# A chunked recurrence on one core: inverse decays by one reciprocal, inputs loaded in three parts, preparation seven slots ahead

## What is computed

```python
for t in range(S):
    y[:, :, t] = np.einsum('bhd,bhde->bhe', rt, state)
    Sa = np.einsum('bhde,bhe->bhd', state, at)
    state_decay = state * wt[:, :, None, :] - np.einsum('bhd,bhe->bhde', Sa, bt)
    state = state_decay + np.einsum('bhd,bhe->bhde', vt, kt)
```

## Time and profile before

| | us |
|---|---|
| median of 3 executions | 1002.68 |
| lowest, highest | 999.1, 1007.23 |
| the profiled execution | 1005.59 |
| its span in the trace | 1003.9 |
| TensorE busy in the span | 826.9 |
| VectorE busy in the span | 556.5 |

### The profile page before, as it was taken

How to read it: one execution, slowest core, us unless ns; L and a number is a source line. 1 busy time by engine, 2 the same in 40 slices (tenths; PEclk the granted TensorE clock), 3 DMA queues, 4 the chain that set the end, 5 groups by cost and what they waited for, 6 DMA issues and landing times.

```text
span 1003.9 us, 27604 instructions
## 1 busy us (share of the span) xinstructions
PE 826.9 (82%) x11872; PEld 603.9 (60%) x11872; DVE 556.5 (55%) x1235; ACT 312.4 (31%) x739; POOL 252.2 (25%) x524
## 2 busy tenths in 40 slices
PE   2318988897998978859998789997899987899977
PEld 2218888897887978844454555455544545554555
DVE  8686667767776653125436635347355366353464
ACT  3102222223222222212225532235422255312354
POOL 1075856687776876000000000000000000000000
PEclk9999787898777888789999999999999999999999
DMA  3525455565656536232000000100000000000000
GB/s 102 137 57 115 96 131 127 131 147 112 137 121 132 133 73 159 60 101 81 10 31 7 21 14 1 40 1 21 14 7 30 10 12 17 14 1 0 1 21 20
DMA packets 125336, 61.31 MB, mean 61 GB/s; under 512 B 105120, under 2 KB 118048, under 8 KB 123296
## 3 DMA queue, kind: packets, MB, share of 16 engines
q1 hardware_dynamic: 95172, 32.61, 14.5%
q10 hardware_dynamic: 30044, 26.94, 10.4%
HBM read 45.37 MB, written 14.16 MB: 59 GB/s over the span
## 4 chain that ended last, share of the span: by engine, by line
PE 66%; DVE 15%; DMA 7%; ACT 6%; issue 4%; SPq 2%; ACTq 1%; DVEq 0%
PE ps_all L737 9%; PE ps_all L721 8%; PE ps_scan L103 4%; PE ps_all L778 4%; DMA l_by_unit<-l_blocks 3%; PE ps_all L854 3%; PE ps_all L815 3%; PE ps_scan L194 3%; ACT probs L914 3%; PE ps_scan L174 3%; PE ps_all L833 3%; PE ps_all L731 3%; PE ps_all L845 2%; PE ps_all L724 2%; DVE t_update_first L314 2%
## 5 line engine op out<-in xcount | busy, mean ns | idle before, releaser
L314 POOL TENSOR_TENSOR t_update<-l_by_unit,t_by_unit 128x133 f32<-128x133 f32 (+13 forms) x251 | 118.0, 470 | 131.8 <-DVE t_by_unit L316 64.4
L316 POOL TENSOR_TENSOR t_by_unit<-t_by_unit,t_update 128x133 f32<-128x133 f32 (+13 forms) x251 | 128.8, 513 | 19.7
L103 PE MATMUL ps_scan<-decayed_a_and_eye,scaled_then_x 40*128 40x104 f32 x768 | 67.8, 346 | 55.9 <-DVE decayed_a_and_eye L346 55.9
L721 PE MATMUL ps_all<-scaled_then_x,inputs_then_w_up 128*128 128x384 f32 x256 | 91.0, 499 | 15.7 <-DMA scaled_then_x<-y_t 10.0
L103 PEld LDWEIGHTS ps_scan<-decayed_a_and_eye,scaled_then_x 40*128 40x128 f32 x768 | 62.7, 252 | 57.9 <-DVE decayed_a_and_eye L346 42.3
L1005 DVE TENSOR_REDUCE minus_max<-ps_all 128x1 f32<-128x128 f32 (+5 forms) x96 | 54.9, 618 | 75.2 <-PE ps_all L819 75.2
L737 PE MATMUL ps_all<-gated,w_down 128*128 128x384 f32 x256 | 91.1, 499 | 0.0
L721 PEld LDWEIGHTS ps_all<-scaled_then_x,inputs_then_w_up 128*128 128x128 f32 x256 | 48.7, 194 | 52.2 <-issue 12.0
L880 ACT ACTIVATE h<-ps_all 128x384 f32<-128x384 f32 x64 | 28.0, 490 | 148.7 <-PE ps_all L724 148.7
L737 PEld LDWEIGHTS ps_all<-gated,w_down 128*128 128x128 f32 x256 | 46.0, 189 | 44.6 <-issue 19.1
L951 DVE TENSOR_SCALAR conv<-h,w_conv 128x768 f32<-128x768 f32 x32 | 19.9, 621 | 94.7 <-ACT h L880 94.7
(11 more groups left out here) (115 smaller groups left out, 1519.2 us busy)
## 6 DMA issues: line engine op xcount, KB each, us to landing
inputs_then_w_up<-in_x ACTq DMA_DIRECT2D x46, 321.4 KB
r_t_and_v_t<-in_rv ACTq DMA_DIRECT2D x48, 160.0 KB
l_by_unit<-l_blocks SPq DMA_DIRECT2D x24, 256.0 KB, 5.0
uv_and_ruv<-in_v ACTq DMA_DIRECT2D x48, 80.0 KB, 3.0
y_t<-y_out SPq DMA_DIRECT2D x24, 160.0 KB
out<-out_rows SPq DMA_DIRECT2D x24, 160.0 KB, 1.8
l_blocks<-ak_and_l SPq DMA_DIRECT2D x96, 32.0 KB, 2.0
t_blocks<-t_by_unit SPq DMA_DIRECT2D x24, 128.0 KB, 4.7
```

Source lines behind the costliest of these rows:

```text
L103: last = nc.tensor.matmul(PS[:, o:o + ROWS], weights, AL[c % NK][rows(h), p, :], start=True, stop=True)
L314: return (lambda: eng.tensor_tensor(tmp[:, 0:cols, 0:rest], l[:, s:s + 1, s + 1:BLK].broadcast_to(shape), t[:, 0:cols, s:s + 1].broadcast_ ...
L316: lambda: eng.tensor_tensor(t[:, 0:cols, s + 1:BLK], t[:, 0:cols, s + 1:BLK], tmp[:, 0:cols, 0:rest], ALU.subtract))
L721: nc.tensor.matmul(bank[n][:, 0:HALF], WIN[:, t, cols], XT[:, t, n * HALF:(n + 1) * HALF], start=(t == 0), stop=False)
```

## The change

Four things change together. (1) `suffixes`, a small reciprocal and a backward scan, becomes `inverses`: one reciprocal of all 104x512 prefix products into a new tile; the tiles of the scan go. (2) The load of a chunk is cut in three: w, then a, then k and b, each with its semaphore; 46 load DMAs become three times as many, each of a part. w of chunk n+8 is loaded after the first move of slot n, a of chunk n+7 after the second, k and b of chunk n+8 after bkn_move. (3) GA goes from 6 to 7: one slot more before slot 0, an eighth `decayed_a_and_eye`, `ak_and_l` and `bk_natural`, a ninth `prefix_products`. (4) The order within a slot: in odd slots with a head VectorE begins with four steps of the head, then hm, then five steps, then gm, and only then prefixes and inverses; ScalarE does the second x move ahead of bkn_move. solve_first stands in slot -3, again behind gm of chunk 3.

```diff
--- before.py
+++ after.py
@@ -20,11 +20,13 @@
 WCOLS = P8 * SEGW
 HC = P8 * C
 XCOLS = WCOLS + 1 + 3 * HC
-GA = 6
+GA = 7
 NK = GA + 1
 NQK = GA + 2
 NPAIR = NT // 2
 HEAD = 9
+FIRST = 4
+PARTS = {"w": slice(0, WCOLS + 1), "a": slice(WCOLS + 1, WCOLS + 1 + HC), "kb": slice(WCOLS + 1 + HC, XCOLS)}
 
 
 def recurrence(nc, sem, in_x, in_v, in_rv, l_dram, t_dram, y_t, inputs, scaled, load_weights, load_tokens):
@@ -35,9 +37,8 @@
     INX = [inputs[0:ROWS, n * XCOLS:(n + 1) * XCOLS] for n in range(2)]
     BK = [scaled[0:ROWS, n * 2 * HC:(n + 1) * 2 * HC].rearrange("r (p j t) -> r p j t", p=P8, j=2) for n in range(2)]
     PF = [sb(f"prefix_products{n}", [ROWS, WCOLS]) for n in range(NQK)]
-    SF = sb("suffix_products", [ROWS, WCOLS + 3])
+    IV = sb("inverse_products", [ROWS, P8, C])
     ONE = sb("reset_ones", [ROWS, WCOLS + 1])
-    RST = sb("reset_inverses", [ROWS, WCOLS + 1])
     AL = [sb(f"decayed_a_and_eye{n}", [ROWS, P8, ROWS]) for n in range(NK)]
     GM = [sb(f"ak_and_l{n}", [128, 2, P8, C]) for n in range(NK)]
     BKN = [sb(f"bk_natural{n}", [128, 2, P8, D]) for n in range(NK)]
...
@@ -244,11 +245,11 @@
                 act.wait_ge(m["t_out"], 32 * (j - 1))
             nc.scalar.activation(TS[j % 2][:, :, :], EYE[:, :, :], ACT.Copy).then_inc(m["eye"], 1)
 
-        def load_x(c):
+        def load_x(c, part):
             if c >= 2:
                 act.wait_ge(m["prepped"], c - 1)
             for h in range(2):
-                act.dma_start(INX[c % 2][rows(h), :], in_x[c, h]).then_inc(m[f"inx{c % 2}"], 16)
+                act.dma_start(INX[c % 2][rows(h), PARTS[part]], in_x[c, h][:, PARTS[part]]).then_inc(m[f"{part}{c % 2}"], 16)
 
         def load_v(n):
             if n >= 3:
@@ -264,7 +265,8 @@
                               in_rv[n, h].rearrange("r k p t -> r (k p t)")).then_inc(m[f"r{n % 3}"], 16)
 
         act.wait_ge(m["set_inx"], 2)
-        load_x(1)
+        for part in ("w", "kb", "a"):
+            load_x(1, part)
         act.wait_ge(m["consts"], 4)
         for n in range(NK):
             for h in range(2):
@@ -277,11 +279,14 @@
         for n in range(-GA, NT + 1):
             c = n + GA - 1
             live, ahead = 0 <= n < NT, 0 <= c < NT
+            soon, next_up = 2 <= n + GA < NT, 2 <= n + GA + 1 < NT
             if live: move(XS, PX, "x", "x_sb", n)
+            if next_up: load_x(n + GA + 1, "w")
             if live: move(YS, PY, "y", "y_sb", n, -1.0)
-            if 2 <= n + GA + 1 < NT: load_x(n + GA + 1)
+            if soon: load_x(n + GA, "a")
+            if live: move(ZS, PX, "e", "z_sb", n)
             if ahead: bkn_move(c)
-            if live: move(ZS, PX, "e", "z_sb", n)
+            if next_up: load_x(n + GA + 1, "kb")
             if live: u_move(n)
             if live:
                 act.wait_ge(m["st"], n + 1)
@@ -319,27 +324,25 @@
     def vector(dve):
 
         def prefixes(c):
-            dve.wait_ge(m[f"inx{c % 2}"], 32 * (c // 2 + 1))
+            dve.wait_ge(m[f"w{c % 2}"], 32 * (c // 2 + 1))
             if c >= 1:
                 dve.wait_ge(m["prepped"], c)
             link(dve, nc.vector.tensor_tensor_scan(PF[c % NQK][:, :], INX[c % 2][:, 0:WCOLS], ONE[:, 0:WCOLS], 0.0,
                                                    ALU.mult, ALU.add))
 
-        def suffixes(c):
-            ends = RST[:, 1:WCOLS + 1].rearrange("r (p w) -> r p w", w=SEGW)[:, :, C]
-            link(dve, nc.vector.reciprocal(ends, pf3(c)[:, :, C]))
-            link(dve, nc.vector.tensor_tensor_scan(SF[:, 1:WCOLS + 1][:, ::-1], INX[c % 2][:, 1:WCOLS + 1][:, ::-1],
-                                                   RST[:, 1:WCOLS + 1][:, ::-1], 0.0, ALU.mult, ALU.add))
+        def inverses(c):
+            link(dve, nc.vector.reciprocal(IV[:, :, :], pf3(c)[:, :, 1:SEGW]))
 
         def bk(c):
+            dve.wait_ge(m[f"kb{c % 2}"], 32 * (c // 2 + 1))
             if c >= 2:
                 dve.wait_ge(m["g"], c - 1)
-            sf = SF[:, 2:2 + WCOLS].rearrange("r (p w) -> r p w", w=SEGW)[:, :, 0:C]
             o = WCOLS + 1 + HC
             nc.vector.tensor_tensor(BK[c % 2], INX[c % 2][:, o:o + 2 * HC].rearrange("r (p j t) -> r p j t", p=P8, j=2),
-                                    sf.unsqueeze(2).broadcast_to([ROWS, P8, 2, C]), ALU.mult)
+                                    IV[:, :, :].unsqueeze(2).broadcast_to([ROWS, P8, 2, C]), ALU.mult)
 
         def al(c):
+            dve.wait_ge(m[f"a{c % 2}"], 32 * (c // 2 + 1))
             if c >= NK:
                 dve.wait_ge(m["x"], c - NK + 1)
             o = WCOLS + 1
@@ -387,13 +390,14 @@
                 else:
                     sub().then_inc(m["solved"], 1)
 
-        def solve_head(j):
-            dve.wait_ge(m["l_in"], 32 * (j + 1))
-            dve.wait_ge(m["eye"], j + 1)
-            dve.wait_ge(m["solved"], 1)
-            if j >= 3:
-                dve.wait_ge(m["head"], j - 2)
-            for s in range(HEAD):
+        def solve_head(j, steps):
+            if steps.start == 0:
+                dve.wait_ge(m["l_in"], 32 * (j + 1))
+                dve.wait_ge(m["eye"], j + 1)
+                dve.wait_ge(m["solved"], 1)
+                if j >= 3:
+                    dve.wait_ge(m["head"], j - 2)
+            for s in steps:
                 mult, sub = step(nc.vector, LU[j % 2], TS[j % 2], TMD, s)
                 link(dve, mult())
                 if s < HEAD - 1:
...
@@ -421,12 +424,20 @@
                 dve.wait_ge(m["consts"], 4)
                 nc.vector.tensor_copy(MK[0:C, :], M0[0:C, 0:C])
                 link(dve, nc.vector.tensor_copy(MK[C:128, :], M0[C:128, C:128]))
-            if prep: prefixes(c)
-            if after: hm(n - 1)
-            if prep: suffixes(c)
-            if n % 2 == 1 and 2 <= (n + GA - 3) // 2 < NPAIR: solve_head((n + GA - 3) // 2)
-            if ahead: gm(g)
-            if n == -2: solve_first()
+            pair = (n + 3) // 2
+            if n % 2 == 1 and 2 <= pair < NPAIR:
+                solve_head(pair, range(0, FIRST))
+                hm(n - 1)
+                solve_head(pair, range(FIRST, HEAD))
+                if ahead: gm(g)
+                if prep: prefixes(c)
+                if prep: inverses(c)
+            else:
+                if prep: prefixes(c)
+                if after: hm(n - 1)
+                if prep: inverses(c)
+                if ahead: gm(g)
+            if n == -3: solve_first()
             if prep: bk(c)
             if 1 <= n and n - 1 < NT - NPAR: state(n - 1)
             if after: y_out(n - 1)
...
```

More of the change, by code:

```diff
@@ L72, in recurrence @@
              "solved pool_chain set_eye consts set_inx set_dve set_pool arrived go "
-             "inx0 inx1 v0 v1 v2 r0 r1 r2 l_out0 l_out1 l_in t_out t_in0 t_in1 stored0 stored1")
+             "w0 w1 a0 a1 kb0 kb1 v0 v1 v2 r0 r1 r2 l_out0 l_out1 l_in t_out t_in0 t_in1 stored0 stored1")
     m = {n: sem("r_" + n) for n in names.split()}
@@ L408, in vector @@
         dve.wait_ge(m["chain"], chain[0])
-        nc.vector.memset(ONE[:, 0:WCOLS].rearrange("r (p w) -> r p w", w=SEGW)[:, :, 0:1], 1.0)
-        link(dve, nc.vector.memset(RST[:, :], 0.0))
+        link(dve, nc.vector.memset(ONE[:, 0:WCOLS].rearrange("r (p w) -> r p w", w=SEGW)[:, :, 0:1], 1.0))
         for x in range(NPAR):
@@ L527, in sync @@
         sp.wait_ge(m["set_inx"], 1)
-        for h in range(2):
-            sp.dma_start(INX[0][rows(h), :], in_x[0, h]).then_inc(m["inx0"], 16)
+        for part in ("w", "kb", "a"):
+            for h in range(2):
+                sp.dma_start(INX[0][rows(h), PARTS[part]], in_x[0, h][:, PARTS[part]]).then_inc(m[f"{part}0"], 16)
         sp.wait_ge(m["set_pool"], 1)
```

## The result

| | before | after |
|---|---|---|
| median, us (executions; of before one more than above) | 1004.95 (4) | 1028.8 (4) |
| lowest to highest, us | 999.1 to 1009.24 | 1022.42 to 1032.89 |
| profiled execution, us | 1005.59 | 1025.99 |
| its span, us | 1003.9 | 1024.3 |

The ratio is 1.0263, with a 95% interval of 1.0209 to 1.0318. The forecast was 983, with a range to 1008: wrong in sign and 46 us off.

What follows compares the result with a forecast made beforehand. TensorE, near full and often at its lower clock, was taken as the bound. Work 184, idle 10.8, new waits 12 and clock 32, less 8, gave 231 us, 23 less; with +4.5 and -3 elsewhere, 983 us, range 956 to 1008.

Steps and rivals of the forecast that it cites:

- the clock's loss: TensorE's steady state: time lost at the lower clock level, up to 48 us before, taken as 32 after.
- new waits: Steady state: idle time from VectorE arriving late, booked at 0.75 us a slot, 12 us over 16 slots.
- What bounds it: Steady state: TensorE is near full; its own work is 11.8 us a slot, against 15.9 measured before.
- the wait of the odd slot: TensorE's 21.7 us ahead of all_blocks in odd slots, taken as gone through earlier l_in and second x move.
- The inverses: VectorE: one 104x512 reciprocal replaces scan and small reciprocal; 0.7 us taken, bounds 0.5 and 2.7, worth nothing by itself.
- Rival D: The reciprocal is slow, 4.4 us a slot on VectorE, so no steady-state gain: about 1010 us, chance 0.05.
- What is late next on VectorE: Odd slots: four head steps wait for eye ahead of hm; 3.6 us against 3, so 0.6 us of TensorE idle.
- Rival C: Head in front of hm waits for `l_by_unit` and eye, delaying g_products and gm: 1021 us, chance 0.08.
- The solve's chain: From head through GpSimd's part (26.1 us, perhaps 25) to first_blocks: a floor of 13.6 or 13.2 us a slot.
- Before the steady state: Prologue: one more slot costs 6.9 us, a smaller load ahead of the solve returns 2.5; net +4.5.
- Three loads: ScalarE issues six DMAs where it issued two, between moves where it waits for TensorE; costed at nothing.
- The sum: Steady state: work 184, idle 10.8, new waits 12, clock 32, less 8: 231 us, 14.4 a slot.

Runs made afterwards that it cites:

- (a): The kernel before with only the large reciprocal of the change in place of the small reciprocal and backward scan: 1012.55 us, ratio 1.0112.
- (b): The changed kernel with the small reciprocal and backward scan put back in place of the large reciprocal: 1016.55 us, ratio 1.0139.

## Why the prediction was wrong

**The steady state in the terms of the sum.** The forecast split the stage from 112 to 366 us into 184 us of work at the upper level, idle time and the clock's loss (here less the 8 us that it took off). What TensorE is busy over 184 is then the clock's:

| 16 slots, us | clock | idle | all |
|---|---|---|---|
| before, from the earlier trace rows | 37.5 | 32.5 | 254 |
| forecast | 24 | 22.8 | 231 |
| after | 44.1 | 25.9 | 254 |

Of the 23 us that were missed, 20 are the clock's term and 3 the idle time's. **This is the step that failed in the slots:** the clock was to be milder "as two thirds of the idle go", but the forecast's own sum let only 9.7 of 32.5 us go, since it booked 12 us of new waits, and 6.6 went. The granted clock stayed at 0.81 where 0.87 was forecast. Why busy time rose by 6.6 us isn't shown; with eye early, idle and busy time fell together.

**What bounds it, and the wait of the odd slot: half right.** Both waits of the earlier trace rows went. But "I take them as gone", as a gain, was not borne out by itself: the move that removes the larger one alone gave 0.5% of 1004.

**The inverses: the term that was sized wrong.** The lower and upper bounds were 0.5 and 2.7 us, 0.7 was taken, and it measured 3.35, outside both. The upper bound took its rate from 1 to 8 columns, where part of the growth is hidden in the fixed time; 6.25 ns from 8 columns on would have given 3.4. The lower one leaned on the difference from an addition, and at the 2.4 ns a column that the text lets pass 512 columns are 1.4 us already. And the sentence that the saving or cost "lies in idle time" holds for the kernel before, where (a) hid the reciprocal in the wait for `l_by_unit`, and not once that wait is gone: the additions put 2.0 us more on VectorE a slot and made it 0.8 us longer ((260.7 - 246.7) / 17), because TensorE waits for items far down VectorE's list, not because its sum was full. Rival D described this but put its price at 7 us over the run.

**What is late next on VectorE: found, and priced too low.** The prediction named eye and gave 3.6 us against 3, so 0.6 us of idle. Both sides of it came from one row. Before, hm starts 0.1 us after the product L166 ends, in every odd slot; eye ends 0.3 us after that product in the row used and 0.8 on average over nine odd slots. After, it is 1.6 on average, hm ends 4.9 us after the product instead of 3.6, and in the slot shown TensorE stands 1.88 us. TensorE's 13 waits ahead of g_products sum to 16.9 us in the stretch, against 12 booked. So the price of the wait itself was missed by 5 us; what was missed beside it is that busy time goes with it, since with eye early 17 slots fell from 264.6 to 245.1, half of it busy time. Rival C had the mechanism, head in front of hm, with `l_by_unit` as its cause; that one landed in time and eye did not. Its price was nearly the result, its chance 0.08, and the nearness is luck: it had neither the reciprocal nor more than 4.5 us for the late slot 0 in it.

**The solve's chain: not the bound in the change.** 25 us for GpSimd's part was close (24.5). Behind slot 0 TensorE didn't wait for the solve's result in the changed kernel, and for 3.0 us in the kernel with scan and early eye, whose slots took 14.4 us. The floor of 13.2 us a slot was neither reached nor refuted.

**Before the steady state: +16.3 against +4.5.** GA = 7 alone cost 9.1, where 6.9 was booked. The 2.5 us for a smaller load did not show: GA = 7 alone, with one load, and (b), with three, have slot 0 at 87.89 and 87.84. The prefix that started at 42.39 now starts at 46.50, behind an al that waited 7.1 us for its own part of the load. With the scan slot 0 starts at 87.84, so the other 7.3 us are the reciprocal's: five of 3.37 us stand in the chain from 0 to 80 us, where two backward scans of 1.25 us stood. The last, at 77.45, stands ahead of gm, for which l_out and behind it t_out wait. This place in SP's queue the prediction did not look at.

**Three loads: booked at nothing, worth about 1.5%** in the kernel with the other faults mended, by the ratios.

**The sum.** 14.4 us a slot is what the scan with the early eye measured, and the whole then took 984 to 988 us. That is partly luck. In the terms above, scaled to 16 slots, this kernel has 32 us of clock and 14.5 of idle, where the forecast had 24 and 22.8: the two errors cancel. And it isn't the change that was forecast, but a kernel with a scan and another order on ScalarE.

## What to carry to other kernels

Take the rate of an instruction from two large sizes, or bound it by the steepest slope seen and then some; a few small columns show the fixed cost, not the rate. When an instruction moves to the head of an engine's list, list every semaphore that it waits for and the time at which each fires, over all slots and not in one: everything behind it inherits the latest of them. An engine that is busy for three quarters of the slot has little slack if another engine waits for the last items of its list. And a gain from the clock that is argued from idle time must use the idle time that the sum itself leaves.

## What the runs showed of the hardware

The reciprocal on VectorE takes about 0.15 us and 6.25 ns a column in float32, with 32 partitions as with 104: 3.35 us for 104x512, eight times an addition of that shape (0.43), and 2.6 times a scan of 104x520 (1.30). With the reciprocal in place of the scan on VectorE, GpSimd's 502 instructions of the solve took 231 to 233 us in four kernels, against 243 to 249 with the scan, and 254 with the scan and four additions beside them. A load of the same bytes in three parts instead of one went with 1.5% less time, and the traces name no cause.
